# Tokens as rows in the last tile's second down product, and two stores of whole rows

## The chip, the cores and the metric

The kernel runs on one NeuronCore of a Trainium2 chip. The metric is the device time of one execution in microseconds. The span of a profile is the time from the first to the last instruction on the core.

## The reference

The input x has 2 x 4096 tokens of 192 channels. A causal convolution over 7 tokens (softmax-normalised taps, one set for each of 8 heads of 24 channels) is followed by two MLPs without biases:

```python
x = attn_out.reshape(B * S, D)                    # 8192 tokens x 192
h = x @ w_in1;  g = where(h >= 1, h, where(h <= -1, 0, (h + 1) ** 2 / 4))
y = g @ w_out1                                    # 192 -> 2048 -> 192
h = y @ w_in2;  g = h / (1 + exp(-1.702 * h))
out = g @ w_out2                                  # 192 -> 2048 -> 192
```

All inputs and the output are fp32.

## The kernel before

The 8192 tokens are cut into 16 tiles of 512 (4 slabs of 128). Partition p holds 64 consecutive tokens of the input, and a slab is one token of each partition. Channels or hidden units lie on the partitions during the MLPs, tokens along the free dimension. The hidden width of 2048 is cut into 16 steps of 128.

Products are made in float32r, with operands split into a high part (rounded) and a low part (what is left), and the three products high x high, high x low and low x high are summed in PSUM. For a down product, w_down holds for each step 384 columns: the 192 of the high part (128 "main", 64 "rest") and then the low part, with its rest columns first and its main columns behind. So the slice 128:256 gives one stationary operand whose lower 64 columns are the rest of the high part and whose upper 64 are the rest of the low part. down2 (L699 to L716) is one step of the second MLP's down product. It has five matmuls, each with 128 stationary columns of weights and 512 moving columns (tokens): w_main, w_lo and w_rest on the high part of the activations (L709, L710, L713), w_main and w_rest on the low part (L715, L716). They fill two banks, acc2, with channels as rows.

The second MLP runs 24 steps behind the first, and its down product 2 more behind that. In the loop and around it both run together in 64-row halves of the array (begin_up, end_up, down_both). After the last step of the first MLP only the second remains: tail_slot then issues, for each step, up2 (five matmuls, L515 to L519, into h[2] or h[3]) and down2 of two steps before. The queues are in order on each engine, and the order is that of the slot functions of each engine. ScalarE makes the high part of the activated h (L804) once TensorE has finished the down product two steps before (g2_hi has two buffers), then the activation again as fp32 (L808); VectorE makes the low part (L982).

The output of a tile leaves like this. take_out (ScalarE, L821 to L826) copies the two banks of acc2 to SBUF. sum_out (VectorE, L1005) adds the two halves of the rest bank. turn_main and turn_rest (L1011, L1016) transpose blocks of 32x32. store (SP, L362) issues 24 transfers of 16 KB (L360), each with runs of 32 channels, 128 bytes, in DRAM. The first down2 of the next tile waits for out_copied before it overwrites the main bank and for out_summed before the rest bank. For the tile before the last this falls into the tail, as do all the steps of the last tile.

The banks h[0], h[1] and acc1 belong to the first MLP, which has left them by then.

Of the kernel before, what the change touches and what calls it, by code (L numbers as in the profile page):

```python
# [6 lines left out]
ALU = mybir.AluOpType  # L7
ACT = mybir.ActivationFunctionType
# [11 lines left out]
def conv_mlp_mlp(nc, x, conv_w, w_in1, w_out1, w_in2, w_out2, out):  # L20
    P = 128
    BATCH, SEQ, D = x.shape
# [3 lines left out]
    SLABS = TOKENS // P  # L26
    SLABS_PER_TILE = 4
# [30 lines left out]


    out_turned = out.rearrange("(b t j) d -> t j b d", j=SLABS, t=TURN)  # L60
    xf = x.rearrange("b s d -> (b s) d").rearrange("(p j) d -> p j d", j=SLABS)

    with ExitStack() as ctx:
# [3 lines left out]
        def sem(name):  # L67
            return ctx.enter_context(nc.semaphore(name))
# [38 lines left out]
        h = [ctx.enter_context(nc.psum_tensor(f"h{k}", [P, 512], FP32)) for k in range(4)]  # L107
        acc1 = [ctx.enter_context(nc.psum_tensor(f"acc1_{k}", [P, 512], FP32)) for k in range(2)]
        acc2 = [ctx.enter_context(nc.psum_tensor(f"acc2_{k}", [P, 512], FP32)) for k in range(2)]

        x_loaded = sem("x_loaded")
        x_halo = sem("x_halo")
# [45 lines left out]
        rest_out_turned = sem("rest_out_turned")  # L158
        main_stored = sem("main_stored")
        rest_stored = sem("rest_stored")  # L160


        act_cols = slice(POOL_HEADS * HEAD_D, (POOL_HEADS + ACT_HEADS) * HEAD_D)
# [148 lines left out]
        @block.sync  # L312
        def _(sp):
            def load_raw(n):
                m = n // N_CHUNKS
                kind, c = CHUNKS[n % N_CHUNKS]
                before = raw_before(n)
                if before is not None and before < DVE_CHUNKS:
                    sp.wait_ge(w_ready, DVE_CHUNKS + before + 1)
                elif before is not None:  # L320
                    sp.wait_ge(wp_ready, before - DVE_CHUNKS + 1)
                w_in, w_out = (w_in1, w_out1) if m == 0 else (w_in2, w_out2)
                done = loaded_of(n)
                cols = slice(c * IN_CHUNK, (c + 1) * IN_CHUNK)
                if kind == "main":
                    sp.dma_start(raw_view(n), w_in[0:DM, cols]).then_inc(done, 16)
                elif kind == "rest":
                    for part in range(2):
                        sp.dma_start(raw_view(n)[part * DR:(part + 1) * DR, :],
                                     w_in[DM:D, cols]).then_inc(done, 16)  # L330
                else:
                    rows = w_out.rearrange("(f p) d -> p f d", p=P)[:, c * OUT_CHUNK:(c + 1) * OUT_CHUNK, :]
                    sp.dma_start(raw_view(n), rows).then_inc(done, 16)

            def load_first(tile):
                j0 = tile * SLABS_PER_TILE
                halo = HALO - j0
                sp.dma_start(x_in[:, halo:, :], xf[:, 0:j0 + SLABS_PER_TILE, :]).then_inc(x_loaded, 16)
                for b in range(BATCH):
                    p0, p1 = b * PARTS_PER_BATCH + 1, (b + 1) * PARTS_PER_BATCH  # L340
                    sp.dma_start(x_in[p0:p1, 0:halo, :],
                                 xf[p0 - 1:p1 - 1, SLABS - halo:SLABS, :]).then_inc(x_halo, 16)

            def load(tile):

                sp.wait_ge(conv_step, tile * CONV_STEPS)
                if isinstance(tile, int) and tile == 2:
                    sp.wait_ge(conv_sum2, TAPS - 1)
                sp.dma_start(x_in[:, :, :],
                             xf[:, bass.ds(tile * SLABS_PER_TILE - HALO, HALO + SLABS_PER_TILE), :]  # L350
                             ).then_inc(x_loaded, 16)

            MAIN_BLOCKS, REST_BLOCKS = DM // TURN, DR // TURN

            def store_blocks(tile, turned, blocks, d0, done):
                for k in range(blocks):
                    d = d0 + k * TURN
                    src = turned[k * TURN:(k + 1) * TURN, :].rearrange("t (j b c) -> t j b c", j=SLABS_PER_TILE, c=TURN)
                    for b in range(P // TURN):
                        sp.dma_start(out_turned[:, bass.ds(tile * SLABS_PER_TILE, SLABS_PER_TILE), b, d:d + TURN],  # L360
                                     src[:, :, b, :]).then_inc(done, 16)

            def store(tile):
                sp.wait_ge(main_out_turned, tile + 1)
                store_blocks(tile, main_turned, MAIN_BLOCKS, 0, main_stored)
                sp.wait_ge(rest_out_turned, tile + 1)
                store_blocks(tile, rest_turned, REST_BLOCKS, DM, rest_stored)

            sp.dma_start(taps[:, :, :].rearrange("p h k -> p (h k)"),
                         bass.AP(tensor=conv_w.tensor, offset=0, ap=[[0, P], [1, HEADS * TAPS]])  # L370
                         ).then_inc(taps_loaded, 16)
            load_first(0)
            for n in range(6):
                load_raw(n)

            sp.wait_ge(xT_ready, 1)
            load_first(1)
            for n in range(6, 12):
                load_raw(n)
            load(2)  # L380
            for n in range(12, 14):
                load_raw(n)
            load(3)
            for n in range(14, 2 * N_CHUNKS):
                load_raw(n)
            with nc.Fori(0, LOOP_PAIRS, engines=(sp.engine,), hint_back_edge=True) as i:
                for tile, side in loop_tiles(i):
                    load(tile + 2)
                    store(tile - 2)
            for tile in range(TILES - 4, TILES):  # L390
                store(tile)
            sp.wait_ge(main_stored, 16 * TILES * MAIN_BLOCKS * (P // TURN))
            sp.wait_ge(rest_stored, 16 * TILES * REST_BLOCKS * (P // TURN))

        @block.gpsimd
        def _(pool):
# [114 lines left out]
        def _(pe):  # L511
# [187 lines left out]
            def down2(step):  # L699

                first, last = step.s == 0, step.s == F_TILES - 1
                w = w_down[1][:, step.s, :]
                hi, lo = g2_hi[step.s % G_RING], g2_lo[step.s % G_RING]
                w_main, w_rest, w_lo = w[:, 0:DM], w[:, DM:DM + 2 * DR], w[:, D + DR:2 * D]
                main, rest = acc2
                pe.wait_ge(g2_hi_ready, step.n + 1)
                if first:
                    pe.wait_ge(out_copied, step.tile * 2 - 1)
                nc.tensor.matmul(main[:, :], w_main, hi[:, :], start=first, stop=False)  # L709
                nc.tensor.matmul(main[:, :], w_lo, hi[:, :], start=False, stop=False)  # L710
                if first:
                    pe.wait_ge(out_summed, step.tile)
                nc.tensor.matmul(rest[:, :], w_rest, hi[:, :], start=first, stop=False)  # L713
                pe.wait_ge(g2_lo_ready, step.n + 1)
                nc.tensor.matmul(main[:, :], w_main, lo[:, :], start=False, stop=last)  # L715
                nc.tensor.matmul(rest[:, :], w_rest, lo[:, :], start=False, stop=last).then_inc(down2_done, 1)  # L716

            def transpose_x(tile, banks):
                pe.wait_ge(conv_step, (tile + 1) * CONV_STEPS)
                if tile == 1:  # L720
                    pe.wait_ge(conv_sum2, TAPS - 1)
                for j in range(SLABS_PER_TILE):
                    tok = slice(j * P, (j + 1) * P)
                    nc.tensor.transpose(banks[0][:, tok], x_conv[:, j, 0:DM], ident[:, :])
                    ins = nc.tensor.transpose(banks[1][:, tok], x_conv[:, j, D - P:D], ident[:, :])
                ins.then_inc(xT_ready, 1)
# [30 lines left out]
            def tail_slot(tile, side, s):  # L757
                n = tile * F_TILES + s
                two = back(tile, side, s, BEHIND)
                if n == ALL_STEPS:  # L760
                    end_up(back(tile, side, s, 1), back(tile, side, s, BEHIND + 1))
                    down_both(back(tile, side, s, LAG), back(tile, side, s, BEHIND + LAG))
                if two is not None:
                    up2(two)
                if n == ALL_STEPS + 1:
                    down1(back(tile, side, s, LAG))
                if n > ALL_STEPS:
                    down2(back(tile, side, s, BEHIND + LAG))

            pe.wait_ge(ident_ready, 2)  # L770
            pe.wait_ge(warm_ready, 1)
# [14 lines left out]
        def _(act):  # L786
# [163 lines left out]
            with nc.Fori(0, LOOP_PAIRS, engines=(act.engine,), hint_back_edge=True) as i:  # L950
                run_body(slot, i)
            run_tail(slot)
            take_out(TILES - 1)

        @block.vector
        def _(dve):
# [189 lines left out]
            with nc.Fori(0, LOOP_PAIRS, engines=(dve.engine,), hint_back_edge=True) as i:  # L1146
                run_body(slot, i)
            run_tail(slot)
            turn_main(TILES - 1)
            sum_out(TILES - 1)  # L1150
            turn_rest(TILES - 1)


_INS = ["x", "weight", "moe_w_in", "moe_w_out", "moe2_w_in", "moe2_w_out"]
# [18 lines left out]
```

## Time and profile before

| | us |
|---|---|
| median of 3 runs | 1237.18 (1235.67 to 1237.49) |
| profiled execution | 1237.26 |
| its span | 1235.4 |
| TensorE busy | 1198.1 (97%) |
| VectorE busy | 890.0 (72%) |
| ScalarE busy | 817.4 (66%) |
| GpSimd busy | 471.3 (38%) |
| mean granted TensorE clock | 0.986 |

Times in rows are microseconds from the start of the span unless marked ns. PE is TensorE's matmuls, PEld its loads of stationary operands, DVE is VectorE, ACT ScalarE, POOL GpSimd, SPq the DMA queue of SyncE. L715 is line 715 of the kernel. The end of a matmul record is modelled and lies behind the start of the next one, so the cost of a matmul in a stream is read from start to start. A granted clock of 1.00 is 2.4 GHz, one of 0.50 is 1.2 GHz.

### The profile page before, as it was taken

Reading aid. Unit: us, or ns where it says so; the run is one execution under the profiler, and the core shown is the slowest. Engines: PE = TensorE matmul, PEld = TensorE weight load, DVE = VectorE, ACT = ScalarE, POOL = GpSimd, SP = SyncE. Lnnn points to the kernel's source line nnn. Section 1 sums busy time; section 2 is a strip of 40 time slices with the busy share of each in tenths; the row PEclk is TensorE's granted clock in tenths of the full one; section 3 lists DMA queues with packets and bytes.
Section 4 is the critical chain, followed back from the end, with each engine's and each line's share of the span. In section 5 each row is a group of like instructions: output and inputs, shape, how many; then the busy total and the mean of one; then the engine's idle time right before and its main releaser. Section 6 shows DMA issues by size and latency. Waiting matters only on the chain.

```text
span 1235.4 us, 25844 instructions
## 1 busy us (share of the span) xinstructions
PE 1198.1 (97%) x9326; PEld 1040.4 (84%) x9326; DVE 890.0 (72%) x1205; ACT 817.4 (66%) x1545; POOL 471.3 (38%) x426
## 2 busy tenths in 40 slices
PE   6998899999999999999999999999999999999995
PEld 3776789888988889888888888888888898888874
DVE  6976769687686867868687786868778596765532
ACT  4865676766757677675766757576676767765542
POOL 5858818054170814408072350906326080000000
PEclk8999999999999999999999999999999999999998
DMA  7221000101010010101001010000101000000001
GB/s 170 73 67 59 1 34 12 35 2 46 1 46 1 10 38 1 46 1 33 15 7 40 1 46 1 15 32 5 43 1 46 2 12 4 3 13 1 14 9 18
DMA packets 63569, 30.87 MB, mean 25 GB/s; under 512 B 56052, under 2 KB 60274, under 8 KB 63472
## 3 DMA queue, kind: packets, MB, share of 16 engines
q1 hardware_dynamic: 63472, 29.40, 9.4%
q8 instruction: 82, 1.34, 0.4%
q14 instruction: 15, 0.12, 0.0%
HBM read 23.09 MB, written 6.29 MB: 24 GB/s over the span
## 4 chain that ended last, share of the span: by engine, by line
PE 89%; POOL 5%; ACT 2%; DVE 2%; DMA 1%; issue 1%; SPq 0%; POOLq 0%; ACTq 0%; DVEq 0%
PE acc L664 6%; PE acc L673 4%; PE h L587 4%; PE h L607 4%; PE acc L675 4%; PE h L605 4%; PE h L589 4%; PE h L609 4%; PE h L585 4%; PE acc L670 4%; PE h L611 4%; PE h L602 4%; PE h L592 4%; PE acc L648 4%; PE acc L667 3%; PE acc L646 3%
## 5 line engine op out<-in xcount | busy, mean ns | idle before, releaser
L804 ACT ACTIVATE g_hi<-h 128x512 fp32r<-128x512 f32 x256 | 153.2, 598 | 172.4 <-PE h L613 145.2
L970 DVE TENSOR_TENSOR gate<-h,clip 128x512 f32<-128x512 f32 x232 | 160.4, 691 | 141.6 <-ACT clip L790 137.6
L790 ACT ACTIVATE clip<-clip,half 128x512 f32<-128x512 f32 x256 | 185.3, 724 | 109.9 <-DVE clip L961 99.9
L961 DVE TENSOR_SCALAR clip<-h 128x512 f32<-128x512 f32 x256 | 175.2, 684 | 97.8 <-PE h L611 94.0
L982 DVE TENSOR_TENSOR g_lo<-gate,g_hi 128x512 fp32r<-128x512 f32 x256 | 215.6, 842 | 34.2 <-ACT gate L808 34.2
L976 DVE TENSOR_TENSOR g_lo<-gate,g_hi 128x512 fp32r<-128x512 f32 x232 | 223.7, 964 | 19.3 <-ACT g_hi L796 5.2
L423 POOL TENSOR_TENSOR x_conv<-x_in,tap_w 128x384 f32<-128x384 f32 (+2 forms) x30 | 26.3, 896 | 510.4 <-ACT raw L844 507.1
L430 POOL TENSOR_TENSOR x_conv<-x_conv,prod 128x384 f32<-128x384 f32 (+2 forms) x180 | 216.2, 1219 | 1.6
L796 ACT ACTIVATE g_hi<-gate 128x512 fp32r<-128x512 f32 x232 | 146.8, 633 | 79.1 <-DVE gate L970 79.1
L423 POOL TENSOR_TENSOR prod<-x_in,tap_w 128x384 f32<-128x384 f32 (+2 forms) x180 | 193.2, 1094 | 7.9 <-DMA x_in<-in_x 3.2
L808 ACT ACTIVATE gate<-h 128x512 f32<-128x512 f32 x256 | 148.6, 580 | 0.0
L666 PE MATMUL acc<-g_hi,w_down 64*128 64x512 f32 x231 | 115.3, 499 | 0.0
L664 PE MATMUL acc<-g_hi,w_down 64*128 64x512 f32 x231 | 113.7, 492 | 0.0
L844 ACT ACTIVATE raw<-x_conv 32x128 f32<-32x128 f32 x336 | 103.3, 307 | 6.2 <-POOL x_conv L430 1.6
L634 PE MATMUL acc<-g_hi,w_down 64*128 64x512 f32 x231 | 91.5, 396 | 2.5 <-ACT g_hi L796 2.5
L664 PEld LDWEIGHTS acc<-g_hi,w_down 64*128 64x128 f32 x231 | 42.4, 184 | 59.7 <-PE acc L656 59.6
L651 PE MATMUL acc<-g_hi,w_down 64*128 64x512 f32 x231 | 92.4, 400 | 0.0
L646 PE MATMUL acc<-g_hi,w_down 64*128 64x512 f32 x231 | 91.8, 398 | 0.0
L658 PE MATMUL acc<-g_lo,w_down 64*128 64x512 f32 x231 | 91.5, 396 | 0.0
L656 PE MATMUL acc<-g_lo,w_down 64*128 64x512 f32 x231 | 91.0, 394 | 0.3 <-DVE g_lo L976 0.2
L654 PE MATMUL acc<-g_hi,w_down 64*128 64x512 f32 x231 | 91.2, 395 | 0.0
L648 PE MATMUL acc<-g_hi,w_down 64*128 64x512 f32 x231 | 91.2, 395 | 0.0
(253 smaller groups left out, 4848.8 us busy)
## 6 DMA issues: line engine op xcount, KB each, us to landing
x_in<-in_x SPq DMA_DIRECT2D x14, 960.0 KB, 4.6
out_y<-raw SPq DMA_DIRECT2D x384, 16.0 KB, 1.4
raw<-in_moe_w_out SPq DMA_DIRECT2D x6, 384.0 KB, 3.3
raw<-in_moe_w_in SPq DMA_DIRECT2D x4, 512.0 KB, 7.5
raw<-in_moe_w_in SPq DMA_DIRECT2D x8, 256.0 KB, 7.3
stage<-in_moe_w_out SPq DMA_DIRECT2D x2, 384.0 KB, 14.7
x_in<-in_x SPq DMA_DIRECT2D x1, 768.0 KB, 4.9
x_in<-in_x SPq DMA_DIRECT2D x2, 283.5 KB
```

What stands on the lines that cost most here:

```text
L423: ins = nc.gpsimd.tensor_tensor(by_head(dst, j), by_head(x_in, at + j), w, ALU.mult)
L430: ins = nc.gpsimd.tensor_tensor(o, o, prod[k % 2][:, j:j + slabs, 0:width], ALU.add)
L648: nc.tensor.matmul(main2, w2_lo[UPPER, :], hi2[UPPER, :], start=False, stop=False)
L664: nc.tensor.matmul(main1, w1_main[UPPER, :], hi1[UPPER, :], start=False, stop=False)
L790: nc.scalar.activation(c, c, ACT.Square, bias=half[:, :], scale=0.5).then_inc(square_ready, 1)
L796: nc.scalar.activation(g1_hi[step.s % G_RING][:, :], gate1_of(step)[:, :], ACT.Copy).then_inc(g1_hi_ready, 1)
L804: nc.scalar.activation(g2_hi[step.s % G_RING][:, :], src, ACT.Gelu_apprx_sigmoid).then_inc(g2_hi_ready, 1)
L808: nc.scalar.activation(gate2[:, :], src, ACT.Gelu_apprx_sigmoid).then_inc(gate2_ready, 1)
L961: nc.vector.tensor_scalar(clip[step.s % 2][:, :], bank1(step)[:, :], -1.0, 1.0, ALU.max, ALU.min).then_inc(clip_ready, 1)
L970: nc.vector.tensor_tensor(gate1_of(step)[:, :], bank1(step)[:, :], clip[step.s % 2][:, :], ALU.max).then_inc(gate1_ready, 1)
L976: nc.vector.tensor_tensor(g1_lo[k][:, :], gate1_of(step)[:, :], g1_hi[k][:, :].bitcast(FP32), ALU.subtract).then_inc(g1_lo_ready, 1)
L982: nc.vector.tensor_tensor(g2_lo[k][:, :], gate2[:, :], g2_hi[k][:, :].bitcast(FP32), ALU.subtract).then_inc(g2_lo_ready, 1)
```

## The change

The steps of the last tile's second down product are issued by a new function. The activations become the stationary operand, a slab of 128 tokens at a time, and the weights the moving one, so a bank has tokens as rows and 384 columns (high and low weights side by side). Four banks are needed: h[0], h[1], acc1[0] and acc1[1]. A step has eight matmuls, four with 384 moving columns on the high part and four with 192 on the low part. At the end ScalarE copies columns 192:384 of each bank to SBUF, VectorE adds them to columns 0:192 in two pieces (the low part has its rest columns first), and SP stores slabs 0 and 1, then 2 and 3, as whole rows. No transposes are made for this tile. The buffers x_conv and prod[0], whose work is over, take the result and the copy.

```diff
+    out_slabs = out.rearrange("(p j) d -> p j d", j=SLABS)
+        last_banks = [h[0], h[1], acc1[0], acc1[1]]
+        last_out, last_low = x_conv, prod[0]
...
-            for tile in range(TILES - 4, TILES):
+            for tile in range(TILES - 4, TILES - 1):
                 store(tile)
-            sp.wait_ge(main_stored, 16 * TILES * MAIN_BLOCKS * (P // TURN))
-            sp.wait_ge(rest_stored, 16 * TILES * REST_BLOCKS * (P // TURN))
+            for j in range(0, SLABS_PER_TILE, 2):
+                sp.wait_ge(slab_summed, 2 * (j + 2))
+                j0 = (TILES - 1) * SLABS_PER_TILE + j
+                sp.dma_start(out_slabs[:, j0:j0 + 2, :], last_out[:, j:j + 2, :]).then_inc(slab_stored, 16)
+            sp.wait_ge(main_stored, 16 * (TILES - 1) * MAIN_BLOCKS * (P // TURN))
+            sp.wait_ge(rest_stored, 16 * (TILES - 1) * REST_BLOCKS * (P // TURN))
+            sp.wait_ge(slab_stored, 16 * SLABS_PER_TILE // 2)
...
+            def last_down2(step):
+
+                first, last = step.s == 0, step.s == F_TILES - 1
+                w = w_down[1][:, step.s, :]
+                hi, lo = g2_hi[step.s % G_RING], g2_lo[step.s % G_RING]
+                pe.wait_ge(g2_hi_ready, step.n + 1)
+                for j, bank in enumerate(last_banks):
+                    nc.tensor.matmul(bank[:, 0:2 * D], hi[:, j * P:(j + 1) * P], w, start=first, stop=False)
+                pe.wait_ge(g2_lo_ready, step.n + 1)
+                for j, bank in enumerate(last_banks):
+                    ins = nc.tensor.matmul(bank[:, 0:D], lo[:, j * P:(j + 1) * P], w[:, 0:D], start=False, stop=last)
+                    if last:
+                        ins.then_inc(slab_done, 1)
+                if not last:
+                    ins.then_inc(down2_done, 1)
...
-                    down2(back(tile, side, s, BEHIND + LAG))
+                    late = back(tile, side, s, BEHIND + LAG)
+                    if late.tile == TILES - 1:
+                        last_down2(late)
+                    else:
+                        down2(late)
...
-            take_out(TILES - 1)
+            for j in range(SLABS_PER_TILE):
+                act.wait_ge(slab_done, j + 1)
+                nc.scalar.activation(last_low[:, j, :], last_banks[j][:, D:2 * D], ACT.Copy).then_inc(low_copied, 1)
...
-            turn_main(TILES - 1)
-            sum_out(TILES - 1)
-            turn_rest(TILES - 1)
+            for j in range(SLABS_PER_TILE):
+                dve.wait_ge(low_copied, j + 1)
+                nc.vector.tensor_tensor(last_out[:, j, 0:DM], last_banks[j][:, 0:DM], last_low[:, j, DR:D], ALU.add
+                                        ).then_inc(slab_summed, 1)
+                nc.vector.tensor_tensor(last_out[:, j, DM:D], last_banks[j][:, DM:D], last_low[:, j, 0:DR], ALU.add
+                                        ).then_inc(slab_summed, 1)
```

## Rows read from the trace of the kernel before

**Rows 1.** The page: span, busy time by engine, and the chain that ended last

```profile
span 1235.4 us, 25844 instructions
PE 1198.1 (97%) x9326; PEld 1040.4 (84%) x9326; DVE 890.0 (72%) x1205; ACT 817.4 (66%) x1545; POOL 471.3 (38%) x426
PE 89%; POOL 5%; ACT 2%; DVE 2%; DMA 1%; issue 1%; SPq 0%; POOLq 0%; ACTq 0%; DVEq 0%
```

**Rows 2.** One tail slot: window, its length, busy time by engine, clock, DMA

```profile
1174.74:1177.07 2.33, 2.33 (x12) 1.87 (x10) 0.69 (x2) 1.09 (x2) 0.00 (x0) 1.00 0.00 0
```

**Rows 3.** Timeline of the end: start, length, engine, line, operation [idle before]

```profile
1219.49 0.40 PE L709 MATMUL acc<-g_hi,w_down 128*128 128x512 f32 x1
...
1220.46 0.19 PEld L715 LDWEIGHTS acc<-g_lo,w_down 128*128 128x128 f32 x1 [0.54 <-DVE g_lo L982]
1220.57 0.19 PEld L716 LDWEIGHTS acc<-g_lo,w_down 128*128 128x128 f32 x1
1220.80 0.40 PE L716 MATMUL acc<-g_lo,w_down 128*128 128x512 f32 x1
1221.23 0.60 ACT L825 ACTIVATE raw<-acc 128x512 f32<-128x512 f32 x1 [1.55 <-PE acc L716]
...
1222.60 11.23 SPq L360 DMA_DIRECT2D out_y<-raw  x24
1223.19 0.70 DVE L1016 STREAM_TRANSPOSE raw<-raw 64x512 f32<-64x512 f32 x1
```

**Rows 4.** Timeline of SyncE's queue, the stores of the tile before the last

```profile
1195.38 12.47 SPq L360 DMA_DIRECT2D out_y<-raw  x24
```

**Rows 5.** Plain fp32 matmuls: timeline row, and the window around it

```profile
17.43 1.13 PE L775 MATMUL h<-gate,ident 128*128 128x512 f32 x2 [0.64 <-DVE prod L1119]
...
17.43:18.56 1.13, 1.13 (x2) 0.30 (x2) 1.10 (x2) 0.27 (x2) 1.13 (x2) 1.00 0.83 174
```

**Rows 6.** Transposes of 128 columns at either clock, timeline and windows

```profile
22.26 0.42 PE L724 MATMUL acc<-ident,x_conv 128*128 128x128 f32 x1
22.47 0.42 PE L725 MATMUL acc<-ident,x_conv 128*128 128x128 f32 x1
...
63.64 0.27 PE L724 MATMUL acc<-ident,x_conv 128*128 128x128 f32 x1
63.75 0.27 PE L725 MATMUL acc<-ident,x_conv 128*128 128x128 f32 x1
...
21.84:23.32 1.48, 1.48 (x7) 1.48 (x8) 0.97 (x2) 0.00 (x0) 0.00 (x0) 0.50 0.09 25
63.36:64.19 0.83, 0.80 (x8) 0.83 (x9) 0.00 (x0) 0.00 (x0) 0.00 (x0) 1.00 0.04 10
```

**Rows 7.** Timeline of the last tile's first down step

```profile
1186.40 0.39 PE L710 MATMUL acc<-g_hi,w_down 128*128 128x512 f32 x1
...
1186.93 0.59 ACT L808 ACTIVATE gate<-h 128x512 f32<-128x512 f32 x1
...
1187.19 0.50 PE L713 MATMUL acc<-g_hi,w_down 128*128 128x512 f32 x1 [0.40 <-DVE raw L1005]
...
1187.99 0.40 PE L515 MATMUL h<-y_hi_b,in_hi 128*128 128x512 f32 x1
```

**Rows 8.** Groups by line and form: count, busy us, mean ns

```profile
L876 ACT ACTIVATE gate<-x_in,tap_w 128x96 f32<-128x96 f32 x6 | 1.8, 360 | 0.0
L861 ACT ACTIVATE w_down<-raw 128x384 fp32r<-128x384 f32 x12 | 5.6, 512 | 2.5 <-DMA raw<-in_moe_w_out 2.5
L1095 DVE TENSOR_TENSOR taps<-taps,tap_red 128x56 f32<-128x56 f32 x1 | 0.2, 217 | 0.0
L970 DVE TENSOR_TENSOR gate<-h,clip 128x512 f32<-128x512 f32 x232 | 160.4, 691 | 141.6 <-ACT clip L790 137.6
```

**Rows 9.** The page's DMA issues: count, KB each, us to landing; the last stores

```profile
x_in<-in_x SPq DMA_DIRECT2D x14, 960.0 KB, 4.6
out_y<-raw SPq DMA_DIRECT2D x384, 16.0 KB, 1.4
raw<-in_moe_w_out SPq DMA_DIRECT2D x6, 384.0 KB, 3.3
...
out_y<-raw SPq DMA_DIRECT2D x24, 16.0 KB, 1.5
```

More of the change, by code:

```diff
@@ L160, in conv_mlp_mlp @@
         rest_stored = sem("rest_stored")
+        slab_done = sem("slab_done")
+        low_copied = sem("low_copied")
+        slab_summed = sem("slab_summed")
+        slab_stored = sem("slab_stored")
         act_cols = slice(POOL_HEADS * HEAD_D, (POOL_HEADS + ACT_HEADS) * HEAD_D)
```

## The prediction

> **What bounds the kernel now.** I read the page first: TensorE is busy 97% of a span of 1235.4 us, and the chain that ended last is 89% PE [rows 1]. So the kernel is bound by TensorE, except where it has nothing left to do. The profiled execution took 1237.26 us, 1.86 us more than its span; it lies 0.08 us above the median of 1237.18, so a change of the span can be read as a change of the time.
>
> The diff acts only behind the loop, so the stretch to read is the tail. From 1184.8 us on there is no first MLP left, and TensorE works in slots of five up matmuls and five down matmuls, all with 512 moving columns. One slot is 2.33 us (window 1174.74 to 1177.07, granted clock 1.00, the 2.4 GHz level) [rows 2], so a matmul costs 0.233 us. The timeline of the end shows the rest [rows 3]: the last matmul starts at 1220.80, ScalarE starts its copy at 1221.23, VectorE turns, sums and turns until 1223.89, and SP issues 24 transfers of 16 KB in 11.23 us, from 1222.60 to 1233.83. From there to 1235.4 SP mostly waits for the last one to land. So 14.6 us of the end hold no matmul, and the issuing of 24 small transfers is what fills them.
>
> **The change, part by part.** The tile before the last is still stored the old way, its 24 issues running from 1195.38 to 1207.85 [rows 4]; SP is free 15 us before the new stores, so nothing is queued in front of them.
>
> *Wide matmuls.* In each of the 16 steps, three 512-column matmuls on the high part become four of 384 columns. No row has 384. By columns alone it is 0.233 x 384/512 = 0.175 us; if the excess of 0.020 us over 512 columns at 2.4 GHz (0.213) is a fixed cost per matmul, it is 0.16 + 0.02 = 0.18. I take 0.18.
>
> *Narrow matmuls.* Two of 512 on the low part become four of 192. Below, 192 columns at the same pace are 0.233 x 192/512 = 0.0875 us. But each needs its own load of 128 columns. After the wait at 1220.46 the load of L715 starts, and the load behind it starts 0.11 us later, which I read as the moment when the matmul takes the array over [rows 3]. So a load that starts with the matmul before it holds the next one to 0.11 us. I take 0.11. Above, the kernel has plain fp32 matmuls of 512 columns that run as two records in 1.13 us at clock 1.00 [rows 5]; less some 0.27 us from the last column to the recorded end (a 128-column matmul is recorded with 0.27 [rows 6]) that is 0.86/512 = 1.67 ns a column, four cycles at 2.4 GHz. 192 columns at that pace are 0.32 us. Between them, the fp32 transposes, the only matmuls with few columns, follow each other by 0.11 us for 128 columns at the 2.4 GHz level and by 0.21 at the 1.2 GHz level [rows 6]: two cycles a column at both. 192 at that pace are 0.16 us.
>
> A step is then 4 x 0.18 + 4 x 0.11 = 1.16 us against 5 x 0.233 = 1.167: about -0.1 us over 14 steps. (The last two steps gain nothing: there TensorE waits for VectorE's low part until 1220.46 [rows 3], and with 4 x 0.18 it arrives at 1219.49 + 0.72 = 1220.21.) The Trainium skill, "TensorE: Matmul & The Clock Gate", "Back-to-back issue gap", gives N/2.4 + 2.5 ns for a warm matmul, 216 ns for 512 columns, where the trace has 233; its section on LDWEIGHTS gives 107 ns for 128 columns, which the 0.11 us bears out and which would bind the narrow ones. By these figures a new step would be, as an estimate, 4 x 0.1625 + 4 x 0.107 = 1.08 us, and the sum 1.2 us lower than mine; I stay with the rows.
>
> *Four banks instead of two.* The first step of the last tile no longer waits for tile 14's copy out of acc2. Before, its third down matmul starts at 1187.19 instead of 1186.63, and the next slot's first at 1187.99 where 1187.33 was possible [rows 7]: 0.66 us lost. ScalarE's two copies still delay its gate to 1187.52, and up2 two slots on needs that bank, so I take 0.66 - 0.25 = 0.4 us as the gain; bounds 0 and 0.66.
>
> *The end.* The first narrow matmul of the last step starts on the array at 1220.57. Its result is there 0.30 us later (between the 0.27 us of 128 columns and 0.40 of 512), ScalarE starts at 1220.90. A copy of 128x192: between 0.36 us for 96 columns and 0.51 for 384 [rows 8], 0.41 us, to 1221.31. VectorE adds 128x128 and 128x64 per slab. It has 0.22 us for 56 columns and 0.69 for 512 [rows 8], 1.04 ns a column, so 0.29 and 0.23, 0.52 a slab, more than a copy: VectorE sets the pace, 1221.34 + 4 x 0.515 = 1223.40. The first transfer leaves after two slabs and is hidden behind the other two. SP issues the second at 1223.43. It has 192 KB in 128 rows of 1,536 bytes. Landing takes 1.4 us for 16 KB (1.5 in the tail), 4.6 for 960 KB [rows 9]: 3.3 ns a KB, hence 1.5 + 0.6 = 2.1 us. Bounds: 1.4, and the 3.3 us of a 384 KB weight load. Behind the landing before there were 0.45 us (the last issue starts at about 1233.5, + 1.45, to 1235.4). Sum: 1223.43 + 2.1 + 0.45 = 1225.98, which is 9.4 us earlier. Gone from the path are two transposes and the 24 issues.
>
> Span: 1235.4 - 9.4 - 0.4 - 0.1 = 1225.5, and with 1.86 us around it 1227.4; less 0.08 for the median, 1227.3. Nothing else moves: the new waits of SP (for the old stores) are long met, and ScalarE's and VectorE's instructions of the end have nothing behind them.
>
> **The rivals.**
> *Narrow matmuls at the fp32 pace.* This is the one that can end on the other side. The place is the four 192-column matmuls of each step; all evidence for one cycle a column is from 512 columns. At 0.32 us, a step is 0.72 + 1.28 = 2.0 us, +0.83 a step, +11.7 over 14 steps. The two last steps lose about 0.5 (2.72 us from one low part to the next against 2.24, the wait being used up), the stall gives its whole 0.66. At the end the fourth narrow matmul comes 0.96 us after the first, ends 0.54 later, then 0.41 + 0.52 + 0.1 + 2.1 + 0.45: the end lies at 1220.57 + 11.5 + 5.1 = 1237.2, time 1239.0 or, against the median, 1238.9. That is +0.14%. The price from which nothing is gained is 0.11 + 9.9/60 = 0.28 us, and from about 0.33 us it is slower by more than 0.2%. For it: the narrow matmuls there are (transposes) do not reach one cycle a column. Against it: those are plain fp32. The Trainium skill, "FP8 and Floating Point Precision", "TensorE Precision Notes", ties the four passes to true FP32 and not to reduced precision, and says nothing of width; no run here has a narrow fp32r matmul.
> *Narrow matmuls at the transposes' pace.* 0.16 us each: +0.2 us over 14 steps = 2.9 us, the end unchanged because of the 0.25 us of slack and because VectorE sets the pace; with 0.2 more from the stall, 1230.0.
> *The gain at the end is smaller.* If the small ScalarE and VectorE operations or the wide rows cost the upper bounds (landing 3.3 us, 0.3 us for each of eight additions plus waits between them), the end comes 2 to 3 us later: 1229.5 to 1230.5. This is faster too.
>
> **How the numbers follow.** My forecast has a chance of 0.48, the fp32 pace 0.30, the transposes' pace 0.15, the smaller gain at the end 0.07. A measurement of this kernel can tell about 0.2%, 2.5 us, from no change. All but the fp32 pace are faster: 0.70. Of the 0.30, 0.17 lie within 2.5 us and 0.13 above 1239.7, since its forecast is only 0.8 us below that edge. The likeliest case by itself reaches from 1224.8 (narrow ones at 0.0875, wide ones at 0.175, the whole stall, landing 1.5) to 1229.5. Without the fp32 pace only 0.70 is held, so the range goes on to 1240.0.
>
> **What would show it.** Right: starts of the narrow matmuls 0.11 us apart and of wide ones 0.18, tail slots still about 2.33 us, no gap near 1186.8, two SP issues at the end, 4 to 5 us from last matmul to the end of the span. Wrong: narrow starts 0.16 or 0.32 us apart (slots of 2.5 or 3.2 us), VectorE additions far over 0.3 us, or a landing of the last transfer over 3 us. The forecast fails above all if TensorE's pace depends on the number of moving columns.

## The result, and the profile after

| | before | changed |
|---|---|---|
| median of 4 runs, us | 1236.43 (1234.23 to 1237.49) | 1223.93 (1223.67 to 1224.21) |
| profiled execution, us | 1237.26 | 1224.05 |
| its span, us | 1235.4 | 1222.2 |
| mean granted clock | 0.986 | 0.994 |

The changed kernel is faster by 1.0%: ratio 0.9901, 95% interval 0.9884 to 0.9918. One run of before, of 25 on the chip that ran again, took 2333.11 us; it is in no ratio and no interval here. The forecast was 1227.3 in a range from 1224.8; the measured time lies 0.9 us below the range and 3.4 us below the forecast.

The page of the changed kernel, span, busy times and the chain that ended last (as [rows 1]):

```profile
span 1222.2 us, 25922 instructions
PE 1194.6 (98%) x9374; PEld 1018.9 (83%) x9374; DVE 889.4 (73%) x1210; ACT 817.7 (67%) x1547; POOL 471.1 (39%) x426
PE 89%; POOL 5%; ACT 2%; DVE 2%; DMA 1%; issue 1%; SPq 0%; DVEq 0%; POOLq 0%; ACTq 0%
```

The timeline of one slot of the last tile in the changed kernel, TensorE's down part; L739 is the wide matmul, L742 the narrow one, L529 and L530 the next up matmuls (L515 and L516 of before):

```profile
1205.20 0.51 PE L739 MATMUL h<-w_down,g_hi 128*128 128x384 f32 x2
1205.55 0.51 PE L739 MATMUL acc<-w_down,g_hi 128*128 128x384 f32 x2
1205.89 0.36 PE L742 MATMUL h<-w_down,g_lo 128*128 128x192 f32 x2
1206.01 0.30 PEld L742 LDWEIGHTS acc<-w_down,g_lo 128*128 128x128 f32 x2
1206.23 0.19 PEld L529 LDWEIGHTS h<-y_hi_b,in_hi 128*128 128x128 f32 x1
1206.34 0.19 PEld L530 LDWEIGHTS h<-y_lo_b,in_hi 128*128 128x128 f32 x1
...
1207.50 0.51 PE L739 MATMUL h<-w_down,g_hi 128*128 128x384 f32 x2
```

The four wide matmuls take 1205.20 to 1205.89, 0.173 us each. Behind them the loads follow each other by 0.11 us (1206.01, one in between, 1206.23, 1206.34), so the four narrow ones take 0.45 us, 0.112 each. The slot is 2.305 us instead of 2.33 [rows 2]. (The prediction has the first MLP end at 1184.8 us. In the trace of before its last matmul, L697, starts at 1164.93, so the prediction's window of one slot is well placed and its 0.233 us a matmul stand.) Neither the fp32 pace nor the transposes' pace is there.

The first down step of the last tile in the changed kernel (as [rows 7]):

```profile
1184.04 0.52 PE L739 MATMUL h<-w_down,g_hi 128*128 128x384 f32 x2
...
1184.81 0.59 ACT L842 ACTIVATE gate<-h 128x512 f32<-128x512 f32 x1
...
1185.46 0.19 PEld L529 LDWEIGHTS h<-y_hi_b,in_hi 128*128 128x128 f32 x1 [0.29 <-ACT gate L842]
```

The stall for tile 14's banks is gone, and in its place TensorE waits for the gate, which the same copies have delayed. The gate ends at 1185.40, and the first load behind the wait starts at 1185.46.

The end of the changed kernel (as [rows 3]), and its DMA view from 1218 us on:

```profile
1217.67 0.30 PEld L742 LDWEIGHTS h<-w_down,g_lo 128*128 128x128 f32 x2 [0.41 <-DVE g_lo L1018]
...
1218.07 0.55 ACT L989 ACTIVATE prod<-h 128x192 f32<-128x192 f32 x2 [1.17 <-PE h L742]
1218.43 0.29 DVE L1187 TENSOR_TENSOR x_conv<-h,prod 128x128 f32<-128x128 f32 x1 [0.81 <-ACT prod L989]
1218.50 0.56 ACT L989 ACTIVATE prod<-acc 128x192 f32<-128x192 f32 x2
1218.64 0.22 DVE L1189 TENSOR_TENSOR x_conv<-h,prod 128x64 f32<-128x64 f32 x1
1218.77 0.28 DVE L1187 TENSOR_TENSOR x_conv<-h,prod 128x128 f32<-128x128 f32 x1
...
1219.21 1.01 SPq L404 DMA_DIRECT2D out_y<-x_conv  x2
...
1219.62 0.21 DVE L1189 TENSOR_TENSOR x_conv<-acc,prod 128x64 f32<-128x64 f32 x1
```

```profile
out_y<-x_conv SPq DMA_DIRECT2D x2, 192.0 KB, 1.9
```

From the last wait of TensorE (1217.67) to the end of the span are 4.53 us, where before had 14.94 (1220.46 to 1235.4). The row of SyncE's queue joins two issues and the pause between them. Narrower windows, 1219.0 to 1219.7 and 1219.7 to 1221, show each:

```profile
1219.21 0.35 SPq L404 DMA_DIRECT2D out_y<-x_conv  x1
...
1219.86 0.35 SPq L404 DMA_DIRECT2D out_y<-x_conv  x1
```

So an issue of 192 KB is recorded with 0.35 us, and 0.30 us of the 1.01 lie between the two, while SP waits for the last sums. From the start of the second issue to the end are 2.34 us.

**Where the time went.** Three marks cut every profile here: T, the start of the last tile's first down matmul; W, the end of TensorE's last wait; E, the end of the span. All code up to T is the same in the two kernels.

| us | T | T to W | W to E | sum from T |
|---|---|---|---|---|
| before | 1186.17 | 34.29 | 14.94 | 49.23 |
| changed | 1184.04 | 33.63 | 4.53 | 38.16 |

So the stretch that the change touches is 11.1 us shorter, and the other 2.1 us of the two spans' difference lie ahead of it. The windows of the first 70 us show a difference there, in the granted clock. Columns of a window: length, busy time of PE, PEld, DVE, ACT and POOL with counts, granted clock, DMA share, GB/s. Before:

```profile
20.00:30.00 10.00, 7.42 (x21) 5.55 (x22) 6.76 (x10) 5.80 (x9) 5.64 (x6) 0.52 0.51 158
60.00:70.00 10.00, 7.46 (x30) 5.82 (x29) 5.60 (x9) 4.53 (x9) 3.03 (x4) 0.83 0.29 99
```

The changed kernel:

```profile
20.00:30.00 10.00, 7.57 (x24) 5.47 (x24) 6.72 (x10) 5.79 (x10) 5.64 (x6) 0.66 0.51 159
60.00:70.00 10.00, 7.44 (x37) 5.91 (x36) 7.03 (x11) 5.59 (x10) 4.15 (x5) 1.00 0.29 99
```

Where the surplus arises can be read from the instructions by which ScalarE makes g_hi, which come in the same order in both kernels. The eleventh and the twenty-first, in before and then in the changed kernel:

```profile
53.73 0.60 ACT L796 ACTIVATE g_hi<-h 128x512 fp32r<-128x512 f32 x1
83.61 0.60 ACT L796 ACTIVATE g_hi<-h 128x512 fp32r<-128x512 f32 x1
...
53.50 0.60 ACT L830 ACTIVATE g_hi<-h 128x512 fp32r<-128x512 f32 x1
81.82 0.60 ACT L830 ACTIVATE g_hi<-h 128x512 fp32r<-128x512 f32 x1
```

The changed kernel is ahead by 0.23 us at the eleventh, by 1.79 at the twenty-first and by 2.13 at T. So little of the surplus goes with the lower clock of the window 20 to 30, and most of it arises around the window 60 to 70.

### The profile page after: what moved, and what is told of

Read it like the earlier page. It is cut to its first block, busy times and chain, and to the rows that moved or that the text cites. A ratio compares the mean times of both kernels' runs of the same rounds, so it can differ in the third digit from the quotient of the medians.

```text
span 1222.2 us, 25922 instructions
## 1 busy us (share of the span) xinstructions
PE 1194.6 (98%) x9374; PEld 1018.9 (83%) x9374; DVE 889.4 (73%) x1210; ACT 817.7 (67%) x1547; POOL 471.1 (39%) x426
## 4 chain that ended last, share of the span: by engine, by line
PE 89%; POOL 5%; ACT 2%; DVE 2%; DMA 1%; issue 1%; SPq 0%; DVEq 0%; POOLq 0%; ACTq 0%
PE acc L678 6%; PE acc L687 4%; PE h L621 4%; PE acc L689 4%; PE acc L684 4%; PE h L601 4%; PE h L619 4%; PE h L623 4%; PE h L616 4%; PE h L599 4%; PE h L603 4%; PE h L625 4%; PE acc L681 4%; PE h L606 4%; PE acc L662 4%; PE acc L660 4%
## 5 line engine op out<-in xcount | busy, mean ns | idle before, releaser
L444 POOL TENSOR_TENSOR x_conv<-x_conv,prod 128x384 f32<-128x384 f32 (+2 forms) x180 | 215.9, 1218 | 1.6
```

The costliest lines, as they stand in the source:

```text
L444: ins = nc.gpsimd.tensor_tensor(o, o, prod[k % 2][:, j:j + slabs, 0:width], ALU.add)
```

## The experiments

Every experiment was profiled; the table behind the last one collects the marks of all but bank_waits, where T itself is moved. bank_waits, copies_first and one_store were executed once, for the profile alone, so they are read by their marks and have no ratio.

**again: is the surplus the change's?** No edit.

> The changed kernel once more, five rounds. Two explanations for a result 2.6 us better than the forecast. A: about 2.1 us of it lies in code that the change leaves alone, in the first 70 us, where the profiled run of before spent about 3.5 us more at the 1.2 GHz level; then the two kernels' own runs differ by such amounts from run to run, and the difference of medians comes out anywhere from 10.5 to 12.5 us. The stretch from the last tile's first down step to the end stays at 38.2 us (49.2 before). B: all of it comes from the change; then the difference is 12.5 us again and the changed kernel's first down step of the last tile lies at 1184.0 us after the start in each profile, 2.1 us earlier than before.

Measured: 1224.20 us median of 5 runs against 1235.29 for before on the same chip, ratio 0.9915 (0.9902 to 0.9929), 11.1 us. T is 1183.49, and from T to the end are 38.2 us again. Before's own runs that enter the ratio reach from 1233.14 to 1237.29. For A; B's fixed 12.5 us and 1184.0 did not come.

**before_again: can the kernel before have an early T?** The kernel before, unchanged.

> The kernel before, unchanged, profiled once more. Over the eleven experiments and the changed kernel, the last tile's first down matmul starts at 1183.5 to 1184.4 us where the window 60 to 70 us has a granted clock of 1.00, and at 1184.9 to 1186.6 where it has 0.83. If that is chance in the first 70 us and not the kernel's text (A), this profile of the kernel before falls into one of these two groups by its clock, and whatever the group, has 34.29 us from there to the last wait and 14.9 us from the wait to the end. If the two kernels differ there (B), it starts at 1186.2 whatever the clock.

Measured: T at 1184.03, 34.28 us to the last wait, 14.99 from there to the end, span 1233.3. The same program that had T at 1186.17 has it at 1184.03, the changed kernel's figure. The 2.1 us are not lost in the same place as above: before_again's eleventh instruction that makes g_hi starts at 52.55 and its twenty-first at 82.43, 1.18 us ahead of the first profile at both, and the other 0.96 us arise behind them. The grouping by the clock of one window was too coarse (0.83 there, and yet 1184.03), but B, one T for each kernel, has fallen. The run against before itself has ratio 1.0001 (0.9991 to 1.0011).

**small_stores: the issuing at the end.**

```diff
-            for j in range(0, SLABS_PER_TILE, 2):
-                sp.wait_ge(slab_summed, 2 * (j + 2))
-                j0 = (TILES - 1) * SLABS_PER_TILE + j
-                sp.dma_start(out_slabs[:, j0:j0 + 2, :], last_out[:, j:j + 2, :]).then_inc(slab_stored, 16)
+            for j in range(SLABS_PER_TILE):
+                sp.wait_ge(slab_summed, 2 * (j + 1))
+                j0 = (TILES - 1) * SLABS_PER_TILE + j
+                for d in range(0, D, TURN):
+                    sp.dma_start(out_slabs[:, j0, d:d + TURN], last_out[:, j, d:d + TURN]).then_inc(slab_stored, 16)
...
```

> The changed kernel, but each slab is stored by six transfers of 32 channels (16 KB, runs of 128 bytes) instead of one half of a whole-row transfer: 24 issues again. If the gain at the end is the issuing (theory of the prediction): the first slab is summed 1.2 us after the last wait, then 24 issues of 0.47 us = 11.2 us and 1.6 us behind them, the end 14 us after that wait against 4.5 us, so +9.4 us. If it is the two transposes, the copies and the size of the transfers instead, at most +3 us.

Its timeline shows SyncE's queue and the last addition:

```profile
1220.24 11.26 SPq L405 DMA_DIRECT2D out_y<-x_conv  x24
...
1220.98 0.21 DVE L1190 TENSOR_TENSOR x_conv<-acc,prod 128x64 f32<-128x64 f32 x1
```

W to E is 14.07 us, +9.54 against the changed kernel's 4.53, as expected of the issuing. The median is 1233.23 us, ratio to before 0.9987 (0.9977 to 0.9996). With 24 issues, nearly all of the gain is gone, although every sum is ready by 1221.2 and no transpose is made. What is left of it at the end, 14.07 us against 14.94, is the earlier first issue: 1.21 us after the last wait instead of 2.14. The same 384 KB take 11.26 us of SyncE's queue in 24 pieces. Seen alone, in the window 1220 to 1220.5, the first of these issues of 16 KB is recorded with 0.35 us, as each of 192 KB is in the changed kernel, so the number of issues costs and not their size. No run has few issues with short runs of 128 bytes, so what the short runs would cost by themselves stays open.

**two_queues: the same from the other side.** The kernel before, with this in place of SP's stores of the rest channels of the last tile:

```diff
+            act.wait_ge(rest_out_turned, TILES)
+            for k in range(DR // TURN):
+                d = DM + k * TURN
...
+                for b in range(P // TURN):
+                    nc.scalar.dma_start(out_turned[:, (TILES - 1) * SLABS_PER_TILE:TILES * SLABS_PER_TILE, b, d:d + TURN],
+                                        src[:, :, b, :]).then_inc(rest_stored, 16)
...
```

> The kernel before, with the last tile's 8 stores of the rest channels issued by ScalarE's queue beside the 16 of the main channels on SP. If the issuing of single transfers bounds the end: 16 x 0.47 = 7.5 us from SP instead of 11.2, -3.7 us. If the transfers themselves or their landing bound it (both queues share the DMA engines): 0 to -1 us.

```profile
1221.28 7.47 SPq L360 DMA_DIRECT2D out_y<-raw  x16
...
1222.61 3.81 ACTq L961 DMA_DIRECT2D out_y<-raw  x8
```

W to E is 11.16 us, -3.8; median 1230.62, ratio 0.9966 (0.9956 to 0.9977). Two queues issue side by side at the pace of one (7.47 us for 16, 3.81 for 8, so 0.47 and 0.48 us an issue, where 24 on SP alone take 11.23), so it was the issuing engine and not the DMA engines that bound the end.

**banks_alone: the banks by themselves.** The kernel before with the last tile's main and rest in acc1. The diff shows TensorE's part; take_out and sum_out read the same banks.

```diff
-                main, rest = acc2
+                own = step.tile == TILES - 1
+                main, rest = acc1 if own else acc2
                 pe.wait_ge(g2_hi_ready, step.n + 1)
-                if first:
+                if first and not own:
                     pe.wait_ge(out_copied, step.tile * 2 - 1)
...
-                if first:
+                if first and not own:
                     pe.wait_ge(out_summed, step.tile)
...
```

> The kernel before, with the last tile's second down product in acc1 instead of acc2 and so without the waits for tile 14's copy; nothing else. The stall of 0.66 us goes, but the next up product then waits for ScalarE's gate. Prediction's step: -0.4 us. From the trace of the changed kernel, where that wait is 0.39 us: -0.3 us. If the banks were the source of the surplus: -1 us or more.

T to W is 33.97 us against 34.29: -0.32, as the trace of the changed kernel had it. The time, 1234.76 (ratio 0.9998, 0.9988 to 1.0007), can't tell it from nothing. Its timeline shows the new wait: ScalarE's gate ends at 1184.90, and the next up matmul, possible from 1184.71, starts at 1184.96. The load behind it starts only at 1185.06, so 0.35 us of the 0.66 are lost again: 0.25 to the gate and 0.10 to the load that has to come first after a wait.

```profile
1183.55 0.39 PE L710 MATMUL acc<-g_hi,w_down 128*128 128x512 f32 x1
...
1184.31 0.59 ACT L809 ACTIVATE gate<-h 128x512 f32<-128x512 f32 x1
...
1184.96 0.50 PE L515 MATMUL h<-y_hi_b,in_hi 128*128 128x512 f32 x1
```

**bank_waits: the waits put back.** The changed kernel with `pe.wait_ge(out_summed, step.tile)` ahead of the first step's wide matmuls.

> The changed kernel, whose first last-tile step waits again for the copy and the sum of tile 14, as before. That sum ends at 1185.01 in the changed kernel's trace, so its first wide matmul would start at 1185.06 instead of 1184.04, and the next slot, which no longer has to wait for the gate, 0.6 us later than now: +0.6 us from there to the end. If the banks do not matter: 0.

```profile
1184.27 0.40 PE L529 MATMUL h<-y_hi_b,in_hi 128*128 128x512 f32 x1
...
1186.55 0.60 PE L741 MATMUL h<-w_down,g_hi 128*128 128x384 f32 x2 [0.95 <-DVE raw L1043]
...
1219.87 0.30 PEld L744 LDWEIGHTS h<-w_down,g_lo 128*128 128x128 f32 x2 [0.40 <-DVE g_lo L1020]
```

T itself is moved here, so I measure from the up part ahead of it: 1184.27 to 1219.87 is 35.60 us, where the changed kernel has 34.79 (1182.88 to 1217.67). That is +0.8 us, a third more than the 0.6 expected. This form of the down product, with its wait ahead of all four banks, would have paid more for the old banks than before did, 0.8 us against the 0.32 that banks_alone gets back.

**low_96 and low_384: what sets a narrow matmul's time.** The narrow matmul with `w[:, 0:D // 2]` and with all of `w`, and the bank's columns to match.

> The changed kernel with 96 moving columns instead of 192 in each narrow matmul (the low part of the activations is left out for channels 96 to 191). If the load of the stationary operand holds a narrow matmul to 0.11 us, nothing changes: slot 2.31 us, time within 1 us of the changed kernel. If the columns set the pace (0.0875 us for 192), 4 x 0.044 us less in each of 14 steps: -2.4 us.

> The changed kernel with 384 moving columns in the matmuls on the low part too (low x low is added, a term that the other kernels leave out). From the changed kernel's trace a wide one is 0.173 us and a narrow one 0.112: 4 x 0.061 = +0.24 us a slot, 2.55 us, +3.4 us over 14 steps. If narrow ones were slower than they look (the cost being in the load), less than +1 us.

The loads in low_96's timeline and a slot of low_384's:

```profile
1196.89 0.30 PEld L742 LDWEIGHTS acc<-w_down,g_lo 128*128 128x128 f32 x2
...
1197.11 0.19 PEld L529 LDWEIGHTS h<-y_hi_b,in_hi 128*128 128x128 f32 x1
...
1197.22 0.19 PEld L530 LDWEIGHTS h<-y_lo_b,in_hi 128*128 128x128 f32 x1
```

```profile
1195.07 0.51 PE L739 MATMUL acc<-w_down,g_hi 128*128 128x384 f32 x2
1195.42 0.51 PE L742 MATMUL h<-w_down,g_lo 128*128 128x384 f32 x2
1195.76 0.51 PE L742 MATMUL acc<-w_down,g_lo 128*128 128x384 f32 x2
1196.11 0.39 PE L529 MATMUL h<-y_hi_b,in_hi 128*128 128x512 f32 x1
```

With half the columns, loads are still 0.11 us apart and T to W is 33.49 us, 0.14 less: 14 steps with 384 fewer columns each cost the same but for 0.01 us a step. The time agrees (1224.82, ratio 0.9912, 0.9895 to 0.9929). With 384, each is 0.173 us and T to W is 36.77, +3.1 us (1227.18, ratio 0.9933, 0.9916 to 0.9949); the slot is 2.545. That is 13 steps of 0.24 and not 14: the first step's share disappears in the wait for the gate, which is 0.17 us there instead of 0.29. So a narrow matmul has a floor of 0.11 us, and columns decide above it. That the floor is the load fits, since each of these matmuls has a load of 128 columns of its own; but no run has fewer stationary columns, or two matmuls on one load, so a fixed cost per matmul of the same size is not ruled out. The Trainium skill, "TensorE: Matmul & The Clock Gate", "LDWEIGHTS (loading the stationary operand)", gives 107 ns for 128 columns; the 0.11 us of the trace agrees. By the formula in its "Back-to-back issue gap" a 384-column matmul would take, as an estimate, 0.1625 us; the trace has 0.173, and the measurement decides.

**copies_first: ScalarE's and VectorE's pace at the end.** VectorE's `wait_ge(low_copied, j + 1)` made `wait_ge(low_copied, SLABS_PER_TILE)`.

> The changed kernel, but VectorE starts to add only when ScalarE has made all four copies. In the changed kernel the first addition starts 0.76 us after the last wait of TensorE and the eight take 1.40 us. If ScalarE's copies overlap (0.25 us apart though recorded with 0.3), the end comes 0.65 us later; if they are 0.41 us apart as the prediction had it, 1.3 us later. With nothing to wait for between additions: if 1.40 us is VectorE's own pace, it stays; if it was waiting for copies, it falls under 1.2 us.

```profile
1218.28 0.55 ACT L989 ACTIVATE prod<-h 128x192 f32<-128x192 f32 x2 [1.17 <-PE h L742]
1218.71 0.56 ACT L989 ACTIVATE prod<-acc 128x192 f32<-128x192 f32 x2
1219.31 0.29 DVE L1187 TENSOR_TENSOR x_conv<-h,prod 128x128 f32<-128x128 f32 x1 [1.48 <-ACT prod L989]
...
1220.50 0.21 DVE L1189 TENSOR_TENSOR x_conv<-acc,prod 128x64 f32<-128x64 f32 x1
```

The last line is the eighth addition. They take 1219.31 to 1220.71, 1.40 us with nothing to wait for, so that is VectorE's own pace, 0.33 us a slab apart though the two records add up to 0.50. Two copies start 0.43 us before the next two, so they are 0.215 us apart; the row of two is 0.55 long, so each is recorded with 0.33. W to E is 5.22 us, +0.69.

**one_store, late_take_out and three_one: can more be had?** one_store makes one transfer of 384 KB after the last addition. late_take_out moves tile 14's copies one slot later on ScalarE (`s == OUT_SLOT + 1`) and the sum to `OUT_SLOT + 3` on VectorE. three_one adds to that a store of three slabs from SP and of the fourth from ScalarE's queue.

> The changed kernel with one transfer of 384 KB after the last addition instead of two of 192 KB. The issue starts where the second one starts now, 2.16 us after the last wait. If the time to land grows with the size of the transfer (3.3 ns a KB, the prediction's slope), +0.6 us at the end; if the two transfers of now share the DMA engines anyway, 0 to +0.3 us.

> The changed kernel, in which ScalarE copies tile 14's banks out one slot later, behind the gate of that slot, and VectorE's sum follows two slots later. The banks are no longer needed by the last tile, so nothing waits for the copies. The stretch from the first wide matmul to the next slot falls from 1.53 to 1.14 us: -0.39 us in the span behind it. Rival: the copies fill ScalarE's idle 1.2 us of that slot exactly and only shift the delay by a slot: 0.

> As late_take_out, and the end is stored as three slabs by SP and the last slab, 96 KB, by ScalarE's queue. The last issue then starts 2.16 us after the last wait as now, with half the bytes: 3.3 ns a KB x 96 = -0.3 us against late_take_out. Rival: the first transfer, now larger and started later, lands last, or the landing does not depend on the size: 0 or later.

```profile
out_y<-x_conv SPq DMA_DIRECT2D x1, 384.0 KB, 2.3
```

```profile
out_y<-x_conv SPq DMA_DIRECT2D x1, 288.0 KB, 2.1
out_y<-x_conv ACTq DMA_DIRECT2D x1, 96.0 KB, 2.1
```

one_store (first fence) has W to E 5.04 us, +0.5: landing takes 2.3 us for 384 KB against 1.9 for 192, 2.1 ns a KB. Its single issue is recorded with 0.35 us too. late_take_out has T to W 33.25 us, -0.38, as expected; the wait for the gate is gone. Its time, 1225.28 (ratio 0.9919, 0.9902 to 0.9936), can't show it. three_one (second fence) keeps the -0.38 but has W to E 4.76 us, +0.2 instead of -0.3: its 96 KB take as long to land as the 288 KB that left 0.34 us earlier. Time 1224.89, ratio 0.9910 (0.9893 to 0.9927). Neither can be told from the changed kernel.

The marks of all profiles, us; "clock" is the granted clock of the windows 20 to 30 and 60 to 70:

| | clock | T | T to W | W to E |
|---|---|---|---|---|
| before | 0.52, 0.83 | 1186.17 | 34.29 | 14.94 |
| before_again | 0.66, 0.83 | 1184.03 | 34.28 | 14.99 |
| two_queues | 0.66, 0.83 | 1184.86 | 34.28 | 11.16 |
| banks_alone | 0.66, 1.00 | 1183.55 | 33.97 | 14.98 |
| changed | 0.66, 1.00 | 1184.04 | 33.63 | 4.53 |
| again | 0.66, 1.00 | 1183.49 | 33.62 | 4.59 |
| small_stores | 0.51, 0.83 | 1185.40 | 33.63 | 14.07 |
| low_96 | 0.53, 0.83 | 1186.49 | 33.49 | 4.52 |
| low_384 | 0.66, 1.00 | 1184.38 | 36.77 | 4.65 |
| copies_first | 0.66, 1.00 | 1184.26 | 33.62 | 5.22 |
| one_store | 0.66, 1.00 | 1183.94 | 33.62 | 5.04 |
| late_take_out | 0.66, 1.00 | 1183.76 | 33.25 | 4.59 |
| three_one | 0.66, 0.83 | 1185.19 | 33.25 | 4.76 |

The last two columns repeat within 0.06 us between kernels that are the same there, while T moves by 3 us and is latest in the three profiles with the lower clock in both windows.

## Why the prediction was right and wrong

The mechanism of the change was right in each part; the time lay outside the range. The step that failed is the first one, the base: "a change of the span can be read as a change of the time", with no term for the 1184 us ahead of the last tile. Besides it, the term "The end" was 1.0 us too long. The forecast for the profiled execution was 1227.4 (1227.3 against the median) and it took 1224.05. The 3.3 us are these:

- **2.1 us: the profile that served as the base.** The sum took the span of that one profile, and with it T = 1186.17, as fixed. The marks show T anywhere from 1183.5 to 1186.5, in before (1186.17 and 1184.03 for the same program) as in the changed kernel and its variants (1183.49 to 1186.49). Before's four runs span 3.3 us, and its median itself fell from 1237.18 to 1236.43 with one more run. The range had no term for it; one more microsecond below would have held the result. In again the two medians are 11.1 us apart, where the forecast has 9.9 and its range reaches to 12.4; so it was in part chance that the first four runs, 12.5 us apart, fell outside. What is shown is that the surplus lies ahead of T and is not a property of the changed kernel. Why T moves stays open: that a longer time at 1.2 GHz in the first 70 us makes it late is what the table suggests, not a test of it, and between the two profiles of before 1.18 us arise ahead of 52.55 and the rest behind 83.61.
- **1.0 us: the step "The end".** It had 5.52 us from W to E, and 4.53 were measured. I added recorded durations where starts count. VectorE's "0.29 and 0.23, 0.52 a slab" is recorded so (0.28 and 0.21), but the additions overlap and follow each other at 0.33 us a slab: 0.66 us less over four slabs. The first addition came 0.12 us earlier than forecast, and transfer and closing took 2.34 us instead of 2.55, landing 1.9 instead of 2.1. The likeliest case's lower bound of 1224.8 took landing at 1.5 but left the additions at their estimate.
- **0.2 us: T to W.** Forecast 33.8, measured 33.63. A wide matmul is 0.173 us, not 0.18; 0.175 by columns alone was the nearer bound. Narrow ones are 0.112, as taken. So the steps gave 0.34 us, not 0.1. The stall gave 0.32, not 0.4: the prediction counted 0.25 us for the delayed gate and left out the 0.10 us of the load behind that wait, a time that it had itself read at 1220.46; bounds 0 and 0.66 held it.

The issuing, which carries the change, was sized right: both experiments on it came within 0.15 us of 9.4 and 3.7 us.

**The rivals.** Narrow matmuls at the fp32 pace (0.32 us, given a chance of 0.30) and at the transposes' pace (0.16 us, a chance of 0.15) are both ruled out by 0.112 us between starts and by low_96. The first was the only reason why the range went up to 1240 us. The evidence against them was in the trace of before: the load behind the wait at 1220.46 that lets its matmul in after 0.11 us [rows 3], and the 512-column matmuls at one cycle a column; what kept them alive were plain fp32 matmuls, another kind. The transposes' 0.11 us for 128 columns, which the prediction read as two cycles a column, is moreover the size of the floor that 96 and 192 columns show, and each transpose has a load of its own as well; so it need not say anything about columns. The smaller gain at the end (a chance of 0.07) went the other way: no term there came out above its estimate.

## What to carry to other kernels

At the end of a kernel count the issues: 24 transfers of 16 KB at 0.47 us each cost 11 us, while the same 384 KB in two transfers of whole rows cost 0.35 us for each issue and 1.9 to land. The layout that makes rows whole needs three more matmuls a step, and as these are narrower the slot is not longer (2.305 us against 2.33). Chains of small operations on one engine are to be summed from start to start, as the trace's records overlap. Cut two profiles at the point where their code parts before crediting a difference to an edit: here 2.1 of 13.2 us of span lay ahead of it. And profile the kernel before twice before its one profile serves as the base of a forecast.

## What the runs showed of the hardware

- With 128 stationary columns, a float32r matmul of 96 or of 192 moving columns takes 0.11 us from start to start, one of 384 takes 0.173 and one of 512 takes 0.233, all at a granted clock of 1.00.
- A copy of 128x192 out of PSUM on ScalarE is recorded with 0.33 us and repeats every 0.215 (copies_first); an addition of 128x128 followed by one of 128x64 on VectorE repeats every 0.33 us although the two are recorded with 0.49 to 0.50.
- SP and ScalarE's queue issue 16 KB stores with runs of 128 bytes side by side at 0.47 and 0.48 us each (16 in 7.47 us, 8 in 3.81). By itself an issue on SP is recorded with 0.35 us for 16 KB (small_stores), 192 KB (changed) and 384 KB (one_store). Two stores that overlap, 288 and 96 KB, both land after 2.1 us.
- The same program reached the same instruction at 1184.03 and at 1186.17 us in two profiles.
